# An attention front in chunk windows, laid out ahead by numpy and run in skewed rounds

## What is computed

```python
chunk, left_ctx, right_ctx = (32, 16, 8)
for c in range(S // chunk):
    l_start, r_end = max(0, c * chunk - 16), min(S, c * chunk + 32 + 8)
    k_full = concatenate([mem_k, k[:, :, l_start:r_end]])     # v_full alike
    scores = q_c @ k_full.T / sqrt(D)
    a = softmax(scores)
    out[:, :, c_start:c_end] = a @ v_full
```

## Time and profile before

| | us |
|---|---|
| median of three runs | 452.27 (449.51 to 452.42) |
| the profiled execution | 449.91 |
| span of its core | 448.1 |
| TensorE busy | 406.3 (91%) |
| VectorE / ScalarE / POOL busy | 279.8 / 271.9 / 81.8 |
| moved by DMA | 65.45 MB in 104,885 packets |

### The profile page before, as it was taken

One profiled execution on the slowest core, in us unless ns is written; L12 is line 12 of the kernel. 1 busy time (PEld: TensorE's weight loads), 2 busy tenths in 40 slices (PEclk: granted clock), 3 DMA queues, 4 the chain that ended last, 5 costly groups with the idle time before them and its releaser, 6 DMA issues.

```text
span 448.1 us, 9777 instructions
## 1 busy us (share of the span) xinstructions
PE 406.3 (91%) x3060; PEld 328.6 (73%) x3060; DVE 279.8 (62%) x592; ACT 271.9 (61%) x587; POOL 81.8 (18%) x215
## 2 busy tenths in 40 slices
PE   3989999999999999985999942999999999999997
PEld 2889898889888988862234302788888888888885
DVE  6578786878687868756800034657657557557551
ACT  5589887889788978641113053655665655655642
POOL 1001110031002100000000029523223233233230
PEclk9999999999999999996799985799999999999999
DMA  6786766676566768695799950011011010110111
GB/s 170 172 207 164 185 166 165 165 179 168 144 161 163 174 152 265 192 406 207 248 391 408 406 223 0 1 48 47 23 47 43 27 47 31 39 47 23 47 47 47
DMA packets 104885, 65.45 MB, mean 146 GB/s; under 512 B 87176, under 2 KB 87432, under 8 KB 104864
## 3 DMA queue, kind: packets, MB, share of 16 engines
q1 hardware_dynamic: 104864, 65.18, 48.2%
HBM read 58.88 MB, written 6.29 MB: 145 GB/s over the span
## 4 chain that ended last, share of the span: by engine, by line
PE 68%; SPq 10%; DVE 7%; DMA 5%; issue 5%; ACT 3%; POOL 1%; DVEq 0%; ACTq 0%; POOLq 0%
PE psum L1089 30%; PE psum L940 8%; PE psum L963 6%; PE psum L1016 5%; PE psum L1103 4%; SPq L345 4%; DMA wraw<-in_moe_w_out_dram 3%; PE psum L856 3%; PE psum L1076 2%; PE psum L950 2%; PE psum L910 2%; DMA qk<-in_k_dram 2%; PE psum L880 1%; PE psum L886 1%; PE psum L893 1%
## 5 line engine op out<-in xcount | busy, mean ns | idle before, releaser
L1089 PE MATMUL psum<-Wh,utH 128*128 128x512 f32 x192 | 77.6, 404 | 0.8 <-DVE utL L818 0.8
L1089 PE MATMUL psum<-Wh,utL 128*128 128x512 f32 x192 | 75.5, 393 | 0.0
L1089 PE MATMUL psum<-Wl,utH 128*128 128x512 f32 x192 | 75.4, 392 | 0.0
L940 PE MATMUL psum<-kG,qT 128*96 128x128 f32 x512 | 71.8, 285 | 3.6 <-ACT kG L508 3.5
L818 DVE TENSOR_TENSOR utL<-psum,utH 128x512 fp32r<-128x512 f32 x48 | 33.1, 691 | 55.8 <-ACT utH L630 55.8
L940 PEld LDWEIGHTS psum<-kG,qT 128*96 128x96 f32 x512 | 60.2, 169 | 9.7 <-issue 6.1
L669 DVE TENSOR_REDUCE nmax<-psum 96x4 f32<-96x512 f32 x64 | 43.8, 684 | 24.3 <-PE psum L940 22.5
L963 PE MATMUL psum<-vw,PT 128*96 128x65 f32 x512 | 53.0, 246 | 0.0
L621 ACT ACTIVATE e_sb<-psum,negmax 128x1024 f32<-128x1024 f32 x24 | 26.8, 1117 | 39.1 <-DVE negmax L827 39.1
L963 PEld LDWEIGHTS psum<-vw,PT 128*96 128x96 f32 x512 | 48.5, 165 | 2.0 <-issue 1.9
L676 DVE TENSOR_TENSOR Z<-psum,nmax 96x512 f32<-96x512 f32 x64 | 43.9, 686 | 2.5
(11 more groups left out here) (134 smaller groups left out, 621.2 us busy)
## 6 DMA issues: line engine op xcount, KB each, us to landing
slot<-in_moe_w_dram SPq DMA_DIRECT2D x7, 2048.0 KB, 12.6
ring<-in_moe_w_dram SPq DMA_DIRECT2D x16, 512.0 KB, 3.4
ring<-in_moe_w_dram SPq DMA_DIRECT2D x4, 2048.0 KB, 11.0
qk<-in_q_dram SPq DMA_DIRECT2D x32, 192.0 KB, 3.7
qk<-in_k_dram SPq DMA_DIRECT2D x32, 192.0 KB, 3.9
out_dram<-o_sb SPq DMA_DIRECT2D x24, 256.0 KB, 2.0
vw<-in_v_dram SPq DMA_DIRECT2D x32, 168.0 KB
slot<-in_moe_w_dram SPq DMA_DIRECT2D x2, 1024.0 KB, 7.7
```

Source lines behind the costliest of these rows:

```text
L940: last = pe.matmul(psum[0:QT, n % 2, t * KEYS:(t + 1) * KEYS], qT[:, pair % 2, hh, tt * QT:(tt + 1) * QT], kG[:, pair % 2, hh, tt, :], sta ...
L1089: last = pe.matmul(psum[:, 6 + p, :], a[:, p, c, :], w[:, c, :], start=(c == 0 and a is utH and w is Wh), stop=(c == FC2 - 1 and w is Wl))
```

## The change

The part up to the experts is written anew; the orders of the experts and of the tiles are kept.

- **Layout by numpy, before the launch.** `laid_out` gives, for each of the G = 16 pairs of heads, q and k already transposed (head 0 in partitions 0 to 63, head 1 in 64 to 127), the keys with memory keys in place of the missing ones at both ends, and v with its column of ones as one 64-row window for each chunk, memory rows first. All weights and constants are laid out as the core's partitions read them, so a partition's row of a transfer is one run of memory. Transposes of q and k, zero rows, masks and `memkT` go.
- **Transfers.** SP issues q and k of a pair as one transfer (128 rows of 6272 bytes), v as one (128 rows of 6240), and 24 pieces of w1 instead of 16 and one whole matrix, two and one in turn. The ring has six slots and `slot_of` has ten.
- **Windows.** POOL copies the 56-key windows of the 24 chunks and the 8 memory keys into kW.
- **Rounds.** Nothing loops at run time: 23 rounds are written out. Round `it` has scores of pair it, transposes of P of pair it − 1, P times V of pair it − 2, and transposes of x of pair it − 3. A unit of work is a whole pair over 768 tokens (128 x 768 elements for VectorE and ScalarE). The batch jobs stand in the rounds in which `batch_at(it, lag)` names a batch: lag 4 logits, 5 column maximum, 6 its spreading, 7 sum and slot product.
- **Products.** Scores and P times V are done for each chunk and head: stationary 64 rows by 32 columns, 64 or 65 moving columns. The output of chunk j lies in partitions 32j to 32j + 31, of head hh in bank hh (scores) or 4 + hh (P times V). The scale 1/8 is in the exponential.
- **Elsewhere.** x of even and odd batches has a tile each, so POOL's copy goes; dispatch weights stand in 24 tiles of 128 tokens, not 32 of 96.

```diff
-def program(nc, q, k, v, mem_k, mem_v, phi, w1, w2, w_in, w_out, g_ln, ident_dram, fold_dram, mask_q, mask_k, out):
+def program(nc, consts, qk_dram, v_dram, w1, w2, w_in, w_out, out):
...
+        (qk, kW, vW, Z, PT, x0, xT, LT, x1, ed), _ = layout(A, [
+            ("qk", [P, 2, S + KW], F32), ("kW", [P, 2, NC, KEYS], F32),
+            ("vW", [P, 2, NC, D + 1], F32), ("Z", [P, 2, T, 2, KEYS], F32), ("PT", [P, T, P], F32),
+            ("x0", [P, T, DM], F32), ("xT", [P, DC, S], F32), ("LT", [P, 2, TH * P], F32),
+            ("x1", [P, T, DM], F32), ("ed", [P, T, NS], F32)])
+        xs = (x0, x1)
...
-        slot_of = list(range(RS + 5)) + [0, 1, 2, 6, 7, 9]
+        slot_of = list(range(RS + 4)) + [0, 1, 2, 6, 7, 9]
...
+        PIECES = RS * DC
+        ITER = G + 7
+
+        def batch_at(it, lag):
+
+            b, r = divmod(it - HP + 1 - lag, HP)
+            return b if r == 0 and 0 <= b < B else None
+
         block = ctx.enter_context(nc.Block())
...
+            def load_qk(g):
+
+                wait(sp, scored, g - 1)
+                sp.dma_start(qk[:, g % 2, :], qk_dram[g]).then_inc(qk_in[g % 2], 16)
+
+            def load_v(g):
+
+                wait(sp, pv_done, g - 1)
+                sp.dma_start(vW[:, g % 2].rearrange("p c d -> p (c d)"), v_dram[g]).then_inc(v_in[g % 2], 16)
+
+            def load_piece(i):
+                e, c = i // DC, i % DC
+                sp.dma_start(ring[:, e, c * F1:(c + 1) * F1], w1[e, :, c * F1:(c + 1) * F1]).then_inc(w_first, 16)
+
+            load_qk(0)
+            load_qk(1)
+            sp.dma_start(fixed[:], consts).then_inc(fixed_in, 16)
+            load_v(0)
+            load_v(1)
+            piece = 0
+            for it in range(G):
+                if it + 2 < G:
+                    load_qk(it + 2)
+                if it >= 2:
+                    load_v(it)
+                for _ in range(2 - it % 2):
+                    load_piece(piece)
+                    piece += 1
+
+            sp.wait_ge(scored, G)
             load_weight(sp, RS)
+            sp.wait_ge(pv_done, G)
             load_weight(sp, RS + 1)
+            sp.wait_ge(slot_mm, B - 1)
             load_weight(sp, RS + 2)
+            sp.wait_ge(lt_mm, 2 * B)
             load_weight(sp, RS + 3)
...
+            for g in range(G):
+
+                pool.wait_ge(qk_in[g % 2], 16 * (g // 2 + 1))
+                wait(pool, scored, g - 1)
+                keys = qk[:, g % 2, S:S + KW]
+                windows = bass.AP(keys.tensor, keys.offset, [keys.ap[0], [CHUNK, NC], [1, WIN]])
+                pool.tensor_copy(kW[:, g % 2, :, NM:KEYS], windows).then_inc(kw_set, 1)
+                pool.tensor_copy(kW[:, g % 2, :, 0:NM],
+                                 qk[:, g % 2, S + KW - NM:S + KW].unsqueeze(1).to_broadcast([P, NC, NM]))\
+                    .then_inc(kw_set, 1)
 
             def stage(i, p):
...
+            for it in range(ITER):
+                if 0 <= it - 2 < G:
+                    act.wait_ge(p_turned, it - 1)
+                    act.activation(PT[:].rearrange("k t q -> k (t q)"),
+                                   psum[:, 2:4, :].rearrange("k a c -> k (a c)")[:, 0:T * P], ACT.Copy)\
+                        .then_inc(p_out, 1)
+                b = batch_at(it, 4)
+                if b is not None:
+                    for h in range(2):
+                        act.wait_ge(lt_mm, 2 * b + h + 1)
+                        wait(act, l_mm, b)
+                        act.activation(LT[:, h, :], psum[:, 2 + h, 0:TH * P], ACT.Copy).then_inc(lt_out, 1)
+                if 0 <= it - 3 < G:
+                    g = it - 3
+                    act.wait_ge(x_turned, g + 1)
+                    if g % HP == 0:
+                        wait(act, lt_mm, 2 * (g // HP))
+                    act.activation(xT[:, g % HP, :], psum[:, 6:8, :].rearrange("d a c -> d (a c)")[:, 0:T * P],
+                                   ACT.Copy).then_inc(xT_out, 1)
+                if it < G:
+                    act.wait_ge(shifted, it + 1)
+                    act.activation(Z[:, it % 2], Z[:, it % 2], ACT.Exp, scale=float(D) ** -0.5).then_inc(exped, 1)
...
+            for it in range(ITER):
+                if it < G:
+
+                    s = psum[:, 0:2, 0:T * KEYS].rearrange("q h (t k) -> q h t k", k=KEYS)
+                    dve.wait_ge(scored, it + 1)
+                    dve.tensor_reduce(nmax[:], s, AX.X, ALU.max).then_inc(maxed, 1)
+                    dve.wait_ge(maxed, it + 1)
+                    wait(dve, p_turned, it - 1)
+                    dve.tensor_tensor(Z[:, it % 2].rearrange("q t h k -> q h t k"), s,
+                                      nmax[:].unsqueeze(3).to_broadcast([P, 2, T, KEYS]), ALU.subtract)\
+                        .then_inc(shifted, 1)
+                b = batch_at(it, 7)
+                if b is not None:
+                    dve.wait_ge(d_exp, b + 1)
+                    wait(dve, dsum_mm, b)
+                    dve.tensor_reduce(esp[:], ed[:].rearrange("t n s -> t s n"), AX.X, ALU.add).then_inc(esp_ready, 1)
+                if 0 <= it - 2 < G:
+
+                    g = it - 2
+                    o = psum[:, 4:6, 0:T * (D + 1)].rearrange("q h (t d) -> q h t d", t=T)
+                    dve.wait_ge(pv_done, g + 1)
+                    dve.tensor_scalar(rsum[:, 0], o[:, :, :, D], 1e-9, None, ALU.add).then_inc(summed, 1)
+                    dve.wait_ge(summed, g + 1)
+                    dve.reciprocal(rsum[:, 1], rsum[:, 0]).then_inc(inverted, 1)
+                    dve.wait_ge(inverted, g + 1)
+                    if g % HP == 0:
+                        wait(dve, slot_mm, g // HP - 1)
+                    dve.tensor_tensor(xs[g // HP % 2][:, :, g % HP * P:(g % HP + 1) * P]
+                                      .rearrange("q t (h d) -> q h t d", h=2),
+                                      o[:, :, :, 0:D], rsum[:, 1].unsqueeze(3).to_broadcast([P, 2, T, D]), ALU.mult)\
+                        .then_inc(x_done, 1)
...
+            for it in range(ITER):
+                if it < G:
+
+                    pe.wait_ge(kw_set, 2 * (it + 1))
+                    wait(pe, shifted, it)
+                    for t in range(T):
+                        for j in range(CPT):
+                            c = CPT * t + j
+                            for hh in range(2):
+                                rows = slice(hh * D, (hh + 1) * D)
+                                last = pe.matmul(psum[j * CHUNK:(j + 1) * CHUNK, hh, t * KEYS:(t + 1) * KEYS],
+                                                 qk[rows, it % 2, c * CHUNK:(c + 1) * CHUNK], kW[rows, it % 2, c, :],
+                                                 start=True, stop=True, skip_group_check=True)
+                    last.then_inc(scored, 1)
+                b = batch_at(it, 4)
+                if b is not None:
+
+                    pe.wait_ge(xT_out, HP * (b + 1))
+                    pe.wait_ge(p_out, min(it - 1, G))
+                    for h in range(2):
+                        for c in range(DC):
+                            last = pe.matmul(psum[c * NS:(c + 1) * NS, 2 + h, 0:TH * P], phis[:, c, :],
+                                             xT[:, c, h * TH * P:(h + 1) * TH * P], start=True, stop=True,
+                                             skip_group_check=True)
+                        last.then_inc(lt_mm, 1)
+                if 0 <= it - 3 < G:
+
+                    g = it - 3
+                    pe.wait_ge(x_done, g + 1)
+                    wait(pe, xT_out, g)
+                    for lag, emptied in ((5, l_out), (6, col_max), (7, d_shift)):
+                        if batch_at(it, lag) is not None:
+                            pe.wait_ge(emptied, batch_at(it, lag) + 1)
+                    b = batch_at(it, 8)
+                    if b is not None:
+                        pe.wait_ge(dsum_out, b + 1)
+                        pe.wait_ge(slot_out, b + 1)
+                    for t in range(T):
+                        last = pe.transpose(psum[:, 6 + t // 4, t % 4 * P:(t % 4 + 1) * P],
+                                            xs[g // HP % 2][:, t, g % HP * P:(g % HP + 1) * P], ident)
+                    last.then_inc(x_turned, 1)
+                if 0 <= it - 2 < G:
+
+                    g = it - 2
+                    pe.wait_ge(p_out, g + 1)
+                    pe.wait_ge(v_in[g % 2], 16 * (g // 2 + 1))
+                    wait(pe, x_done, g)
+                    for t in range(T):
+                        for j in range(CPT):
+                            for hh in range(2):
+                                rows = slice(hh * KEYS, (hh + 1) * KEYS)
+                                last = pe.matmul(psum[j * CHUNK:(j + 1) * CHUNK, 4 + hh, t * (D + 1):(t + 1) * (D + 1)],
+                                                 PT[rows, t, j * CHUNK:(j + 1) * CHUNK], vW[rows, g % 2, CPT * t + j, :],
+                                                 start=True, stop=True, skip_group_check=True)
```

(72 more changed lines are left out.)

614 lines of the change are left out of this document (112 added, 502 removed).

## The result

| | before | after |
|---|---|---|
| median, us | 451.53 of 4 | 396.52 of 4 (395.04 to 401.4) |
| ratio | | 0.878, 95% interval 0.872 to 0.884 |
| profiled execution / its span | 449.91 / 448.1 | 401.4 / 399.6 |
| last scores end | 191.4 | 127.5 (forecast 97.7) |
| first expert product starts | 214.15 | 165.48 (forecast 129.3) |

The kernel is 12% faster: inside the range, but 31.5 us behind the forecast of 365. The profiled execution was the longest of its four, 1.6% above the shortest; a second profile of the same kernel (after_again, span 395.2) is given beside it where a size rests on it: last scores to 123.7, first expert product at 159.8, 235.4 from there to the end.

What follows compares the result with a forecast made beforehand. TensorE's stream was taken to bind, not the transfers: last scores end at 97.7 us, plus 31.6 run-out gives 129.3, plus 233.95 gives span 363.3, so 365 us; forecast 352 to 378 (chance 0.50), range 350 to 430.

Steps and rivals of the forecast that it cites:

- The end behind the experts: From the first expert product to the end: order and sizes kept, so 233.95 us as before.
- The start and the other engines: First q and k ready at 7.0 us; VectorE 3.7 us a round, POOL 1.6; none of the other engines binds.
- The products: TensorE's work before the last scores: 20 ns a small record, 1.92 us a step of 96, plus transposes, logits and slots.
- The 11 ns from eight queued esp products: Bound below for a small record, from the sum over esp: 1.06 us a step; doubted for 96 in sequence.
- The waits: TensorE's pauses between groups of products before round 15's scores: 0.3 us a round, 4.5 us in all.
- 2 for the slow first rounds: At the start, the first rounds' products run slower than later ones: 2 us added.
- 2 for coupling: Before the last scores, TensorE and transfers are not smooth, with q, k and v only two deep: 2 us added.
- Rival 1: Small records on TensorE are supplied slower than the tiles could take them, 25 to 40 ns each: 380 to 427 us; chance 0.26.
- Rivals 2 and 4: 2: tiles hardly overlap, 81 ns a record gives 553 us, chance 0.09; 4: transfers slower, 300 GB/s gives 387 us, 0.06.
- Rival 3: Thin tiles bring TensorE's granted clock to 0.50 throughout, 35 ns a record, transposes double: 436 us; chance 0.07.
- The run-out: From the end of the last scores to the first expert product: 14.8 us plus 16.8 us of dispatch chain, 31.6 us.

Runs made afterwards that it cites:

- late_pieces: Changed kernel with all 24 w1 weight pieces loaded behind the rounds instead of during them: 389.81 us.
- pieces_one: Changed kernel with one w1 piece loaded in each round and the other eight behind the last v: 388.42 us, ratio 0.860.
- written-out repetition: Changed kernel with the scores of round 8 made eight times more, as written-out copies: 421.44 us.
- scores_diag: pieces_one with only the scores as block-diagonal products for both heads, five ring slots and 20 early pieces: 382.5 us, ratio 0.853.
- scores_diag_late: scores_diag with a w1 piece only in every second round and twelve behind the last v: 380.43 us, ratio 0.842.
- block_diag: Changed kernel with scores and P times V as block-diagonal products for both heads, v in two transfers, 20 early pieces: 405.68 us, ratio 0.900.
- the kernel with v in halves: pieces_one with v of each pair in two transfers of 64 partitions, one behind the other: 414.73 us, ratio 0.923.

## Why the prediction was right in direction and 31 us off

**The end behind the experts: right.** 234.1 us for 233.95 (235.4 in the second profile). Where the expert products start still decides everything.

**The start and the other engines: right.** First scores at 7.07 for 7.0; POOL's large copy 1307 ns; VectorE's maximum over 768 elements 957 ns for 0.95. None of them bound the front: TensorE waited 3.2 us for VectorE and POOL behind the first q and k.

**The products: right in sum, by errors that cancel.** The forecast gave TensorE 53.8 + 1.9 (steps) + 16.9 + 5.7 + 3.1 + 0.8 = 82.2 us of work up to the last scores; the window shows 84.25. But the steps took 24.2 + 20.3 = 44.5 for 55.7, since a record costs 16 ns on average (2784 of them), 12 in an undisturbed step, and not 20. The 11 ns from eight queued esp products were the better row, and the doubt that they would not hold over 96 was wrong. The transposes took 16.1 + 12.6 = 28.7 for 16.9: six cost 0.82 to 0.88 us in some groups and up to 1.54 in others, where the clock is low, where I had 0.65 from a row of eight. Slot products took 6.1 for 3.1. (The lines overlap a little, so their busy times add to more than the 84.25.) That the sum came out right is luck.

**The waits: the step that failed.** "Waits between groups: 0.3 a round, from the 0.20 pauses" made 4.5 us; with 2 for the slow first rounds and 2 for coupling it was 8.5. The trace has 36.25. That difference, 27.7, and the 2 of the products are the 29.8 us by which the last scores are late in that execution; the run-out adds 6.4. It was 5 us longer than the median. In the second profile idle time is 33.6, 25.1 over the forecast, the products 0.9 over, the last scores 26.0 late, and the run-out, 36.2 us, adds 4.5. In either one the waits are over nine tenths of the miss up to the last scores. The 0.20 us came from a kernel whose front was a loop at run time; the change list said that nothing loops any more, and I costed that edit at nothing.

**Rival 1** had the right cause, a stream of small records supplied too slowly, and its 25 to 40 ns hold for the supply as a mean, 29 ns. Its form was wrong. I put it as a pace of every record (2.4 us or more a step would show it), so a reader of the timeline who sees 1.17 us a step would have struck it out. It comes as blocks of 256 instructions at full pace with a stop between, and it reaches only those stretches that eat a block faster than the next arrives. At its lower end, 25 ns, it gave 380 us, and 396.5 lies between that and its 427.

**Rivals 2 and 4: fell.** The tiles overlap, and the 12 ns a record, below the 20 worked out for four column groups alone, say that row groups do too. The transfers did move less than 405 GB/s, 291 at a share of 0.81, which would be 359 at full share, but TensorE waited for them 1.1 us. What harm they did was indirect: with less traffic beside them the pauses and TensorE's busy time were shorter (late_pieces, pieces_one). **Rival 3** happened in part: the clock fell in stretches with pauses (0.50 with TensorE busy 10.22 of 19 us in the written-out repetition) and made transposes dearer. It goes with TensorE's idle time and is not only a matter of the pauses: with 15.0 us of them the clock of the front was 0.97 and 0.92 (scores_diag, scores_diag_late), and with 2.5 but 31 us of waiting for POOL 0.88 (block_diag).

**The run-out**, 38.0 us for 31.6: pauses of 2.03 and 0.50 us are in it too, one group of six transposes cost 1.51, and batch 3's slot product 3.61 for 2.65, at a mean clock of 0.78.

## What to carry to other kernels

Count instructions before unrolling: here a written-out stretch on TensorE needed more than about 3.7 us of work for each 256 instructions (matmul records and weight loads, 128 pairs), or it stopped at the ends of most blocks; a loop body of 192 instructions didn't. Fewer and wider products can then be no slower, and perhaps a little faster (0.853 for 0.860), even when each step costs more and half of its numbers are zeros. A price for gaps taken from a loop says nothing on the same work written out, and a transfer should not be cut into halves of the partitions to get there.

## What the runs showed of the hardware that I had not expected

- A block of 256 TensorE instructions, written out, arrives every 3.46 to 4.02 us with idle transfer engines and a granted clock of 0.50; work goes on 1.37 to 1.50 us behind the end of its packet; the pauses are 1.42 to 3.56 us there, up to 5.2 in the kernel with v in halves.
- Products of 64 rows by 32 columns with 64 moving columns, 4-byte, keep up 12.8 ns a record with its weight load, over 864 in a row. The 25 ns that the Trainium skill gives as the least distance of starts (TensorE: Matmul & The Clock Gate, Part 1) don't bound them. Products of 128 by 32 with 128 columns take 1.52/48 = 32 ns.
- With v, some 38% of the bytes, in transfers of 64 partitions, the transfer engines were busy about a quarter longer for the same bytes; a packet of v took 429 ns instead of 301, and 411 when two queues issued the halves.

**What stays open.** No kernel kept the whole front as a loop with these small products, so what the pauses cost in total is an estimate from their sum. Nor was it shown by what route traffic adds to the pauses (the instruction packet itself takes about 1.05 us in either case), or why the row of pauses began with one of 3.56 us.
